# Gate and value products of the dense layer in seven half-width block products for two rounds of three

## The chip, the cores and the metric

The kernel runs on one core of a Trainium2 chip. TensorE multiplies matrices, VectorE, ScalarE and GpSimd work element by element, and DMA queues move data between the main memory and the on-chip memory SBUF. TensorE writes its sums into PSUM, eight banks of 512 fp32 words for each of 128 partitions. The metric is the device time of one execution in microseconds, lower is better.

## The reference

Three layers follow each other: attention with a mask of hash buckets, a mixture of 8 experts with one expert per token, and a gated dense layer. The change touches the last one alone:

```python
n_tokens, d_model, d_ff = (1536, 512, 1536)

rms = np.sqrt(np.mean(x * x, axis=-1, keepdims=True) + 1e-06)
xn = x / rms * rms_g
g = xn @ w_gate
silu = g * (1.0 / (1.0 + np.exp(-g)))
val = xn @ w_val
return (silu * val @ w_out).astype(np.float32)
```

## The kernel before

All large products are made in three bf16 parts: an operand is split into an upper part (its rounded or cut bf16) and a lower part (what is left), and each product is upper by upper, upper by lower and lower by upper. A tile of fp32 words in SBUF serves as its own upper part through its upper halfwords, which are read at a stride of two.

The dense layer runs in 36 steps: three rounds (`ROUNDS`) of 512 tokens (`GROUP`), and in each round 12 steps (`KF2`), one per block of 128 hidden features. Steps count from 0, so round one has steps 0 to 11. In a step `gate_and_value(n)` makes on TensorE the gate block and the value block, [128 features x 512 tokens] each, over a depth of 512 (four chunks of 128): 2 x 4 x 3 = 24 matmuls of 512 columns (L826 to L828), gate into bank 2(n%2), value into bank 2(n%2)+1. So banks 0 to 3 hold two steps in turn, and step n waits for `sv` of step n-2. `project(n-2)` follows: the hidden block of two steps ago times the output weights, four token tiles of three matmuls of 512 columns (L836 to L838) into banks 4 to 7, where they gather over a whole round.

Between the two lies a chain on the other engines, which VectorE writes as follows:

```python
V.tensor_tensor(gp[n % 2][:, :], bank(2 * (n % 2)), inv_at[:, c, :], ALU.mult).then_inc(gp_ready, 1)
dve.wait_ge(sig_ready, n + 1)
V.tensor_tensor(silu[n % 2][:, :], gp[n % 2][:, :], sig[n % 2][:, :], ALU.mult).then_inc(silu_ready, 1)
```

`inv_at` is one over the token's norm, spread over the partitions. ScalarE makes the sigmoid (L1032). VectorE multiplies with the value bank (`sv`, L1346), ScalarE copies `sv` to bf16 (`s_hi`, L882, a line of a helper that all plain copies share), GpSimd subtracts (`s_lo`, L1463). The projection reads `s_hi` and `s_lo`, of which there are three buffers each. The missing factor of the value, the same norm, is applied in `take_rows`, where ScalarE scales the finished output rows (L1025); GpSimd stores them with an indirect DMA. That is done after each round, in steps 13 and 25 and at the end.

In steps 2 and 5 ScalarE scales and GpSimd splits a further group of gate and value weights (L973, L1422), and in round one GpSimd splits the output weights (L1443). Each engine's queue runs in the order in which the code is written, with semaphores between them; there is no scheduler. The last steps are written out: behind the last `gate_and_value` two tiles of the projections 33 and 34, then the wait for the last `s_lo`, then the rest.

Of the kernel before, what the change touches and what calls it, by code (L numbers as in the profile page):

```python
# [55 lines left out]
OUT_AHEAD = 2  # L56

# [77 lines left out]
def tiles_taken(h, t):  # L135

    return T * h + t + 2 + min((h + 1) // 2, PAIRS - 1)

# [9 lines left out]
def build(nc, qk, v, proj, w_router, w1, w2, w_gate, w_val, w_out, rms_g, consts, out):  # L148
# [14 lines left out]
    with ctx:  # L163
# [59 lines left out]
        unused = sb("unused", [P, TT], F32, at)  # L223
        assert at[0] <= nc.sbuf_usable_end, at
# [37 lines left out]
        gp = [sb(f"gp{i}", [P, GROUP], F32, at) for i in range(2)]  # L262
        sig = [sb(f"sig{i}", [P, GROUP], F32, at) for i in range(2)]
        silu = [sb(f"silu{i}", [P, GROUP], F32, at) for i in range(2)]
        sv = [sb(f"sv{i}", [P, GROUP], F32, at) for i in range(2)]
        gram = [ring[c][:, GWORDS:GWORDS + GROUP].rearrange("p (t c) -> p t c", c=P) for c in range(ROUNDS)]
        o_bufs = [x[:, :] for x in o_sb] + [ring[3][:, GWORDS:GWORDS + DM]]
# [18 lines left out]
        w_low = [group_of(x) for x in low]  # L286

# [93 lines left out]
        gv_ready = sem("gv_ready")  # L381
        gp_ready = sem("gp_ready")
        sig_ready = sem("sig_ready")
# [171 lines left out]
        def _(pe):  # L555
# [276 lines left out]

            def project_tile(n, t):
# [27 lines left out]
            for n in range(2, STEPS):  # L861
                gate_and_value(n)
                if n < STEPS - 1:
                    project(n - 2)


            for n in (STEPS - 3, STEPS - 2):
                pe.wait_ge(slo_ready, n + 1)
                for t in range(2):
                    project_tile(n, t)  # L870
            pe.wait_ge(slo_ready, STEPS)
            for t in range(2):
                project_tile(STEPS - 1, t)
            for t in range(2, GT):
                for n in (STEPS - 3, STEPS - 2, STEPS - 1):
                    project_tile(n, t)
# [3 lines left out]
        def _(act):  # L880
# [126 lines left out]
            nc.scalar.activation(unused[:, :], mean[:, :], ACT.Sigmoid)  # L1007
# [8 lines left out]
            def take_rows(c, t):  # L1016
                i = GT * c + t

                if c < ROUNDS - 1:
                    act.wait_ge(projected, GT * (KF2 * c + KF2 - 1) + t + 1)  # L1020
                else:
                    act.wait_ge(finished, t + 1)
                if i >= len(o_bufs):
                    act.wait_ge(o_stored[i % len(o_bufs)], 16 * (i // len(o_bufs)))
                nc.scalar.activation(o_bufs[i % len(o_bufs)], bank(4 + t), ACT.Copy, scale=inv[:, i:i + 1])\  # L1025
                    .then_inc(o_copied, 1)
# [24 lines left out]
        def _(dve):  # L1051
# [282 lines left out]
            for n in range(STEPS):  # L1334
                c = n // KF2
                dve.wait_ge(gate_half, n + 1)
                dve.wait_ge(inv_ready, c + 1)
                V.tensor_tensor(gp[n % 2][:, :], bank(2 * (n % 2)), inv_at[:, c, :], ALU.mult).then_inc(gp_ready, 1)  # L1338
                dve.wait_ge(sig_ready, n + 1)
                V.tensor_tensor(silu[n % 2][:, :], gp[n % 2][:, :], sig[n % 2][:, :], ALU.mult).then_inc(silu_ready, 1)  # L1340
# [5 lines left out]
                V.tensor_tensor(sv[n % 2][:, :], bank(2 * (n % 2) + 1), silu[n % 2][:, :], ALU.mult).then_inc(sv_ready, 1)  # L1346
# [3 lines left out]
        def _(pool):  # L1350
# [103 lines left out]

            def store_rows(c, t):
# [5 lines left out]
            for n in range(STEPS):  # L1461
                pool.wait_ge(shi_ready, n + 1)
                G.tensor_tensor(s_lo[n % 3][:, :], sv[n % 2][:, :], s_hi[n % 3][:, :], ALU.subtract).then_inc(slo_ready, 1)  # L1463
# [32 lines left out]
```

## Time and profile before

| | us |
|---|---|
| median of 3 runs | 714.94 |
| lowest, highest | 713.0, 716.01 |
| the profiled execution | 717.1 |
| its span, first to last instruction | 715.3 |

Busy in the span: TensorE 655.4 us (92%), VectorE 371.5, ScalarE 297.9, GpSimd 405.1. Matmuls are pipelined, so a matmul's own duration (379 ns for 512 columns) is longer than its distance to the next one; for what a row of matmuls costs, the distances between their starts are to be read. The attention takes the time to about 235 us, the experts to about 414, and the dense layer the rest.

### The profile page before, as it was taken

What the parts mean: (1) busy time and instruction counts of PE and PEld (TensorE: products, weight loads), DVE (VectorE), ACT (ScalarE), POOL (GpSimd) and SP (SyncE); (2) the same over time, 40 slices, a digit from 0 to 9 for tenths busy, and PEclk for the clock granted to TensorE, in tenths of its full rate; (3) what the DMA queues carried; (4) which work ended last, traced back from release to release, by engine and by line L of the source; (5) the groups of instructions that cost most, each with busy time, mean ns of one, the idle gap of its engine ahead of it and who ended that gap; (6) DMA issues with size and microseconds to landing.
All of it is one profiled execution on the core that took longest, in us unless ns stands there. A gap on an engine that the chain in (4) does not pass through costs nothing.

```text
span 715.3 us, 14977 instructions
## 1 busy us (share of the span) xinstructions
PE 655.4 (92%) x6360; PEld 425.5 (59%) x6370; DVE 371.5 (52%) x658; ACT 297.9 (42%) x506; POOL 405.1 (57%) x246
## 2 busy tenths in 40 slices
PE   3899999999998459999999789999999999999997
PEld 0256666666676459999999774444444444444442
DVE  6778888898973844554456544332222222222321
ACT  1355655655655036766668844131131111221112
POOL 5278768777878487998889955553131111131112
PEclk8699999999999689999998679999999999999999
DMA  6985576585396169776778990000000000010001
GB/s 169 244 196 121 150 199 124 132 213 117 75 312 262 45 193 255 283 285 238 238 275 299 310 352 4 1 0 1 0 33 27 0 1 1 0 60 1 0 1 59
DMA packets 59427, 94.38 MB, mean 132 GB/s; under 512 B 30208, under 2 KB 34432, under 8 KB 58336
## 3 DMA queue, kind: packets, MB, share of 16 engines
q1 hardware_dynamic: 57440, 87.12, 41.9%
q0 software_dynamic: 1920, 6.31, 2.3%
q8 instruction: 50, 0.82, 0.5%
q14 instruction: 17, 0.14, 0.1%
HBM read 76.98 MB, written 6.30 MB: 116 GB/s over the span
## 4 chain that ended last, share of the span: by engine, by line
PE 76%; DVE 12%; DMA 3%; POOL 3%; ACT 2%; issue 2%; another core or an unknown queue 1%; SPq 1%; POOLq 0%; DVEq 0%; ACTq 0%
PE psum L828 9%; PE psum L826 9%; PE psum L827 9%; PE psum L836 4%; PE psum L837 4%; PE psum L838 4%; PE psum L591 3%; PE psum L755 3%; PE psum L756 3%; PE psum L774 3%; PE psum L757 3%; PE psum L775 3%; PE psum L776 3%; PE psum L605 3%; PE psum L606 2%; DVE psum L1116 2%
## 5 line engine op out<-in xcount | busy, mean ns | idle before, releaser
L1463 POOL TENSOR_TENSOR s_lo<-sv,s_hi 128x512 bf16<-128x512 f32 x36 | 41.7, 1157 | 197.2 <-ACT s_hi L882 197.0
L1381 POOL TENSOR_TENSOR probs_lo<-probs 128x768 bf16<-128x768 f32 x80 | 118.6, 1491 | 61.1 <-ACT probs L920 60.7
L1415 POOL TENSOR_TENSOR low<-ring 128x4096 bf16<-128x4096 f32 x19 | 132.9, 7016 | 16.2 <-DMA ring<-in_moe_w 16.2
L920 ACT ACTIVATE probs<-psum 128x384 f32<-128x384 f32 x192 | 92.6, 490 | 72.6 <-PE psum L606 70.0
L828 PE MATMUL psum<-y,low 128*128 128x512 bf16 x288 | 109.2, 379 | 0.0
L827 PE MATMUL psum<-y,ring 128*128 128x512 bf16 x288 | 109.1, 379 | 0.0
L826 PE MATMUL psum<-y,ring 128*128 128x512 bf16 x288 | 109.1, 379 | 0.0
L1338 DVE TENSOR_TENSOR gp<-psum,inv_at 128x512 f32<-128x512 f32 x36 | 24.9, 691 | 149.7 <-PE psum L828 145.8
L1116 DVE TENSOR_REDUCE psum<-psum 128x1 f32<-128x768 f32 x96 | 88.5, 960 | 15.2 <-PE psum L591 14.5
L1032 ACT ACTIVATE sig<-gp 128x512 f32<-128x512 f32 x36 | 22.7, 630 | 137.7 <-DVE gp L1338 137.7
L774 PE MATMUL psum<-hT,ring 128*128 128x0 bf16 x320 | 68.6, 234 | 4.0 <-POOL low L1415 2.5
L625 PE MATMUL psum<-value,probs 128*128 128x73 bf16 x576 | 69.1, 199 | 3.1 <-POOL probs_lo L1381 2.1
L626 PE MATMUL psum<-value_lo,probs 128*128 128x72 bf16 x576 | 69.0, 195 | 0.0
L627 PE MATMUL psum<-value,probs_lo 128*128 128x73 bf16 x576 | 69.0, 197 | 0.0
L775 PE MATMUL psum<-hT,ring 128*128 128x0 bf16 x320 | 68.5, 234 | 0.0
L776 PE MATMUL psum<-hT,low 128*128 128x0 bf16 x320 | 68.5, 234 | 0.0
L1289 DVE SCALAR_TENSOR_TENSOR hT<-psum,hT 128x512 bf16<-128x512 f32 x80 | 53.7, 689 | 26.8 <-ACT hT L939 25.7
L605 PE MATMUL psum<-head 128*128 128x384 bf16 x192 | 65.0, 338 | 0.8 <-ACT probs L920 0.4
L606 PE MATMUL psum<-head 128*128 128x384 bf16 x192 | 64.2, 334 | 0.0
L625 PEld LDWEIGHTS psum<-value,probs 128*128 128x128 bf16 x576 | 56.0, 97 | 10.8 <-POOL probs_lo L1381 2.9
L591 PE MATMUL psum<-head 96*128 96x384 bf16 x192 | 51.0, 349 | 11.4 <-DVE psum L1116 9.0
L626 PEld LDWEIGHTS psum<-value_lo,probs 128*128 128x128 bf16 x576 | 56.8, 99 | 6.5
(202 smaller groups left out, 1496.8 us busy)
## 6 DMA issues: line engine op xcount, KB each, us to landing
ring<-in_moe_w SPq DMA_DIRECT2D x20, 2048.0 KB, 8.7
pair_in<-in_qk SPq DMA_DIRECT2D x8, 1152.0 KB, 5.8
head<-in_qk SPq DMA_DIRECT2D x16, 384.0 KB
head<-in_qk SPq DMA_DIRECT2D x32, 192.0 KB, 5.3
head<-pair_in SPq DMA_DIRECT2D x32, 192.0 KB, 3.7
value<-in_v SPq DMA_DIRECT2D x16, 192.0 KB, 5.6
ring<-in_moe_w_gate SPq DMA_DIRECT2D x4, 768.0 KB, 9.5
ring<-in_moe_w_val SPq DMA_DIRECT2D x4, 768.0 KB, 10.8
```

What stands on the lines that cost most here:

```text
L625: mm(o, p_hi, value_up[b][:, kt, :], start=(kt == 0), stop=False)
L626: mm(o[:, 0:VW], p_hi, value_lo[b][:, kt, :], start=False, stop=False)
L774: mm(o, w_hi, hh, start=(f == 0), stop=False)
L775: mm(o, w_hi, hl, start=False, stop=False)
L776: last = mm(o, w_lo, hh, start=False, stop=(f == KF - 1))
L826: mm(o, w_up[g][:, a, j, cols], yh, start=(j == 0), stop=False)
L827: mm(o, w_up[g][:, a, j, cols], yl, start=False, stop=False)
L828: last = mm(o, w_low[g][:, a, j, cols], yh, start=False, stop=(j == KD - 1))
L920: nc.scalar.activation(probs[h % 2][:, t, half * HALF:(half + 1) * HALF], bank(ST_BANK + n % 2)[:, 0:HALF], ACT.Exp, scale=SCALE).then_inc ...
L1116: V.reduce_max(row_max[:, t // 2, t % 2:t % 2 + 1], psum[:, first:first + 2, 0:HALF], AX.XY).then_inc(s_free, 1)
L1381: G.tensor_tensor(probs_lo[par][:, t, :], probs[par][:, t, :], probs_up[par][:, t, :], ALU.subtract)\
L1415: G.tensor_tensor(low[k % RING][:, :], ring[k % RING][:, :], upper[k % RING][:, :, 1], ALU.subtract)\
```

## The change

In rounds two and three the product of [gate; value] with the tokens is cut into blocks: two row blocks (gate, value), two halves of the depth (two chunks of 128 each), two halves of the 512 tokens. Eight products of such blocks become seven, by the scheme of Strassen and Winograd: each is a sum of weight blocks times a sum of token blocks, and the four results are sums of products. Round one works as before, except that the silu is one activation (`Silu`) and VectorE's product falls away.

- **TensorE.** `seven_blocks(n)` makes seven products of 2 x 3 matmuls over 256 columns (`SUB`), 42 in all: product 1 (`crossed`) into half of bank 0, products 2 and 3 into bank 1, 4 and 5 into bank 2, 6 and 7 into bank 3. Each step uses the same banks. It waits for copies and joins of the step before (`blocks_copied`, `blocks_taken`). Between steps 11 and 12 the projections 9 and 10 stand together, and none stands between steps 12 and 13.
- **ScalarE.** `copy_blocks(n)` takes product 1 into both middle quarters of `gv` (512 elements), product 2 and product 4 into a quarter each (256). Then silu, `s_hi` and the step's job.
- **VectorE.** `join_blocks(n)` adds and subtracts the other products into `gv`: five instructions of 512, 256, 512, 256 and 512 elements with one operand in PSUM, then `sv`, now with both operands in SBUF.
- **Jobs.** The sums of weights and of tokens are made beforehand, one job a step in steps 1 to 20, through one buffer `mix`: VectorE makes fp32 sums (weights: 512, 512 and 256 elements; tokens, 8 jobs of a quarter each: 512, 512, 128, 256 and 256), ScalarE the upper parts (1024 and 256; 1024), GpSimd the lower parts. The norm is multiplied into the tokens there, so the later rounds' rows of output need no scale. Weights of feature block f are made in step `WEIGHT_AT[f]`, the tokens of rounds two and three in steps `COLUMN_AT`. They are written where their sources stood, or where round one's tokens stood. A job's sums wait for the lower parts of the job before.
- **Rows of output.** A fourth tile of its own takes the place of a piece of the weights' tile. At the end, tile 2 of the projections 33 and 34 stands ahead of the wait for the last `s_lo`.

```diff
+WEIGHT_AT = [1, 3, 5, 7, 9, 10, 11, 12, 14, 16, 18, 20]
+COLUMN_AT = [2, 4, 6, 8, 13, 15, 17, 19]
...
+            def seven_blocks(n):
+
+                c, f, m = n // KF2, n % KF2, n - KF2
+                if c == 1:
+                    pe.wait_ge(mix_low, job_of_weights(f) + 1)
+                if f == 0:
+                    pe.wait_ge(mix_low, job_of_columns(4 * c - 1) + 1)
+                left, right = slice(0, SUB), slice(SUB, GROUP)
+                if m:
+                    pe.wait_ge(blocks_copied, COPIES * (m - 1) + 1)
+                else:
+                    pe.wait_ge(sv_ready, KF2 - 1)
+                crossed(bank(0)[:, left], c, f, B_CROSS).then_inc(blocks_ready, 1)
+                if m:
+                    pe.wait_ge(blocks_copied, COPIES * (m - 1) + 2)
+                    pe.wait_ge(blocks_taken, TAKES * (m - 1) + 1)
+                plain(bank(1)[:, left], c, f, 1, B_STEP)
+                mixed(bank(1)[:, right], c, f, C_STEP, B_UPPER).then_inc(blocks_ready, 1)
...
-            for n in range(2, STEPS):
+            for n in range(2, KF2):
                 gate_and_value(n)
+                project(n - 2)
+            project(KF2 - 2)
+            seven_blocks(KF2)
+            for n in range(KF2 + 1, STEPS):
+                seven_blocks(n)
                 if n < STEPS - 1:
                     project(n - 2)
...
             for n in range(STEPS):
-                act.wait_ge(gp_ready, n + 1)
+                if n < KF2:
+                    act.wait_ge(gp_ready, n + 1)
+                else:
+                    copy_blocks(n)
+                    act.wait_ge(blocks_taken, TAKES * (n - KF2 + 1))
                 if n >= 2:
-                    act.wait_ge(silu_ready, n - 1)
-                nc.scalar.activation(sig[n % 2][:, :], gp[n % 2][:, :], ACT.Sigmoid).then_inc(sig_ready, 1)
+                    act.wait_ge(sv_ready, n - 1)
+                nc.scalar.activation(silu[n % 2][:, :], gp[n % 2], ACT.Silu).then_inc(silu_ready, 1)
...
-                copy(s_hi[n % 3][:, :], sv[n % 2][:, :]).then_inc(shi_ready, 1)
+                copy(s_hi[n % 3][:, :], sv[n % 2]).then_inc(shi_ready, 1)
                 if n in SPLIT_AT:
                     scale_group(SPLIT_AT.index(n) + 2)
+                if n in WEIGHT_AT:
+                    weights_high(WEIGHT_AT.index(n))
+                if n in COLUMN_AT:
+                    columns_high(COLUMN_AT.index(n))
...
+            def mix_weights(f):
+
+                g, cols = f // GF, slice((f % GF) * P, (f % GF + 1) * P)
+                if job_of_weights(f):
+                    dve.wait_ge(mix_low, job_of_weights(f))
+                dve.wait_ge(w_scaled, KD * (g + 1))
+                w = group_of(ring[g])[:, :, :, cols]
+                V.tensor_tensor(mix[:, 0:4 * P].rearrange("p (a j c) -> p a j c", a=2, j=2), w[:, :, 0:2, :], w[:, :, 2:4, :], ALU.add)
...
+            for n in range(STEPS):
+                if n < KF2:
+                    gate_and_value(n)
+                else:
+                    join_blocks(n)
+                if n in WEIGHT_AT:
+                    mix_weights(WEIGHT_AT.index(n))
+                if n in COLUMN_AT:
+                    mix_columns(COLUMN_AT.index(n))
...
+                if n in WEIGHT_AT:
+                    weights_low(WEIGHT_AT.index(n))
+                if n in COLUMN_AT:
+                    columns_low(COLUMN_AT.index(n))
```

ScalarE's queue from step 12 to step 14, before: a sigmoid and an `s_hi` per step, and in step 13 the four rows of output.

```order
L1032 ACTIVATE sig_161<-gp_159 128x512
L882 ACTIVATE s_hi_149<-sv_165 128x512
L1032 ACTIVATE sig_162<-gp_160 128x512
L882 ACTIVATE s_hi_150<-sv_166 128x512
L1025 ACTIVATE o_sb_155<-psum,inv 128x512
```

The same place after the change, from the silu of step 12 to the copies of step 14 (L999 is the helper for copies; `ring`, `low` and `y` hold the sums):

```order
L1186 ACTIVATE silu_162<-gv_160 128x512
L999 ACTIVATE s_hi_150<-gv_160 128x512
L999 ACTIVATE ring_107<-mix 128x4x256
L999 ACTIVATE low_111<-mix 128x2x128
L999 ACTIVATE gv_161<-psum 128x512
L999 ACTIVATE gv_161<-psum 128x256 x2
L1186 ACTIVATE silu_163<-gv_161 128x512
L999 ACTIVATE s_hi_151<-gv_161 128x512
L999 ACTIVATE y<-mix 128x4x2x128
L1143 ACTIVATE o_sb_156<-psum,inv 128x512
```

The upper parts of the step's job stand behind `s_hi` and ahead of the next step's copies, and in step 13 the rows of output stand behind the job. VectorE's queue in one of these steps, before: three instructions per step.

```order
L1338 TENSOR_TENSOR gp_160<-psum,inv_at 128x512
L1340 TENSOR_TENSOR silu_164<-gp_160,sig_162 128x512
L1346 TENSOR_TENSOR sv_166<-psum,silu_164 128x512
```

And after the change, in step 13 (a job of tokens) and, by its first lines, in every step from 12 on:

```order
L1544 TENSOR_TENSOR gv_161<-gv_161,psum 128x512
L1547 TENSOR_TENSOR gv_161<-gv_161,psum 128x256
L1549 TENSOR_TENSOR gv_161<-gv_161,psum 128x512
L1551 TENSOR_TENSOR gv_161<-gv_161,psum 128x256
L1553 TENSOR_TENSOR gv_161<-gv_161,psum 128x512
L1555 TENSOR_TENSOR gv_161<-gv_161,silu_163 128x512
L1516 TENSOR_TENSOR mix<-y 128x512
L1517 TENSOR_TENSOR mix<-mix,inv_at 128x512
L1519 TENSOR_TENSOR mix<-mix 128x128
L1520 TENSOR_TENSOR mix<-mix 128x256
```

Three instructions became six with five of them joins, and a job's sums stand between `sv` and the next step's joins.

## Rows read from the trace of the kernel before

**Rows 1.** Windows: busy PE, PEld, DVE, ACT, POOL (instructions), granted clock, DMA share, GB/s.
```profile
449.00:701.50 252.50, 252.50 (x1160) 112.55 (x1159) 69.62 (x98) 48.86 (x77) 61.86 (x54) 1.00 0.02 9
```

**Rows 2.** Timeline of TensorE in one step: start, duration, engine, line, operation.
```profile
563.28 0.38 PE L826 MATMUL psum<-y,ring 128*128 128x512 bf16 x1
...
568.46 0.39 PE L836 MATMUL psum<-wo,s_hi 128*128 128x512 bf16 x1
...
571.13 0.38 PE L826 MATMUL psum<-y,ring 128*128 128x512 bf16 x1
```

**Rows 3.** Timeline of the other engines in the same step.
```profile
568.76 0.69 DVE L1346 TENSOR_TENSOR sv<-psum,silu 128x512 f32<-128x512 f32 x1 [0.61 <-PE psum L828]
569.49 0.63 ACT L882 ACTIVATE s_hi<-sv 128x512 bf16<-128x512 f32 x1 [2.06 <-DVE sv L1346]
570.19 1.16 POOL L1463 TENSOR_TENSOR s_lo<-sv,s_hi 128x512 bf16<-128x512 f32 x1 [6.69 <-ACT s_hi L882]
```

**Rows 4.** Timeline of TensorE, token norms of 128 columns, thirteen starts.
```profile
420.78 0.22 PE L801 MATMUL psum<-y 128*128 128x128 bf16 x1
...
421.45 0.22 PE L801 MATMUL psum<-y 128*128 128x128 bf16 x1
```

**Rows 5.** Timeline of the weight loads in the expert stage, neighbours.
```profile
382.02 0.10 PEld L774 LDWEIGHTS psum<-hT,ring 128*128 128x128 bf16 x1
382.10 0.10 PEld L775 LDWEIGHTS psum<-hT,ring 128*128 128x128 bf16 x1
```

**Rows 6.** Groups by shape: count, busy us, mean ns, then idle time before.
```profile
L882 ACT ACTIVATE y<-psum 128x512 f32 x36 | 20.4, 592 | 16.2 <-PE psum L776 15.9
L920 ACT ACTIVATE probs<-psum 128x384 f32<-128x384 f32 x192 | 92.6, 490 | 72.6 <-PE psum L606 70.0
L882 ACT ACTIVATE s_hi<-sv 128x512 bf16<-128x512 f32 x36 | 22.7, 630 | 74.1 <-DVE sv L1346 74.1
L882 ACT ACTIVATE even_window<-xT 128x1536 bf16 x2 | 3.0, 1486 | 0.0
L1346 DVE TENSOR_TENSOR sv<-psum,silu 128x512 f32<-128x512 f32 x36 | 24.9, 692 | 19.6 <-PE psum L828 19.5
L1150 DVE TENSOR_TENSOR x_head<-psum,rden 128x384 f32<-128x384 f32 x16 | 8.9, 558 | 0.5
L1331 DVE TENSOR_TENSOR ring<-cst,inv 128x512 f32<-128x512 f32 x3 | 1.9, 686 | 0.0
L1463 POOL TENSOR_TENSOR s_lo<-sv,s_hi 128x512 bf16<-128x512 f32 x36 | 41.7, 1157 | 197.2 <-ACT s_hi L882 197.0
L1415 POOL TENSOR_TENSOR low<-ring 128x4096 bf16<-128x4096 f32 x19 | 132.9, 7016 | 16.2 <-DMA ring<-in_moe_w 16.2
```

**Rows 7.** Timeline: VectorE with both operands in SBUF beside GpSimd.
```profile
60.89 0.96 DVE L1183 TENSOR_TENSOR probs_lo<-probs 128x768 bf16<-128x768 f32 x1
61.76 2.33 DVE L1093 TENSOR_TENSOR pair_in<-pair_in 128x768 bf16<-128x768 f32 x1
...
61.49 1.68 POOL L1381 TENSOR_TENSOR probs_lo<-probs 128x768 bf16<-128x768 f32 x1 [1.15 <-ACT probs L920]
...
191.87 2.34 DVE L1093 TENSOR_TENSOR pair_in<-pair_in 128x768 bf16<-128x768 f32 x1
...
439.69 0.69 DVE L1346 TENSOR_TENSOR sv<-psum,silu 128x512 f32<-128x512 f32 x1
...
449.76 1.87 DVE L1340 TENSOR_TENSOR silu<-gp,sig 128x512 f32<-128x512 f32 x1 [0.70 <-ACT sig L1032]
```

**Rows 8.** Timeline of TensorE in the tail, around the wait for the last s_lo.
```profile
704.31 0.38 PE L838 MATMUL psum<-wo_lo,s_hi 128*128 128x512 bf16 x1
704.79 0.40 PE L836 MATMUL psum<-wo,s_hi 128*128 128x512 bf16 x1
```

**Rows 9.** Waits of TensorE in the expert stage; windows, columns as in rows 1.
```profile
PE psum L774 <- POOL low L1415: 2.5, 1, 2.5
...
388.00:392.00 4.00, 2.88 (x57) 2.64 (x58) 4.00 (x8) 3.74 (x8) 4.00 (x1) 0.59 0.90 328
272.00:276.00 4.00, 2.50 (x32) 2.36 (x31) 1.31 (x2) 0.60 (x2) 4.00 (x2) 1.00 1.14 206
276.00:280.00 4.00, 4.00 (x51) 4.00 (x49) 0.69 (x1) 4.00 (x3) 4.00 (x1) 1.00 1.10 150
```

More of the change, by code:

```diff
@@ L137, in tiles_taken, with job_of_weights, job_of_columns @@
     return T * h + t + 2 + min((h + 1) // 2, PAIRS - 1)
+def job_of_weights(f):
+    return f + sum(n < WEIGHT_AT[f] for n in COLUMN_AT)
+def job_of_columns(i):
+    return i + sum(n < COLUMN_AT[i] for n in WEIGHT_AT)
 def item_of_hidden(u):
@@ L286, in build, with mixed_high, mixed_low, cross @@
         w_low = [group_of(x) for x in low]
+        mixed_rows = [x[:, 0:GWORDS].bitcast(BF16).rearrange("p (r c) -> p r c", r=2 * KD)[:, 2:6, :] for x in ring]
+        low_rows = [x[:, 0:GWORDS].rearrange("p (r c) -> p r c", r=2 * KD) for x in low]
+        def mixed_high(f):
+            g, i = f // GF, f % GF
+            return mixed_rows[g][:, :, i * 2 * P:(i + 1) * 2 * P]
+        def mixed_low(f):
+            g, i = f // GF, f % GF
+            tail = low[g][:, GWORDS:ITEM] if i == 2 else ring[g][:, GWORDS + 512 * i:GWORDS + 512 * (i + 1)].bitcast(BF16)
+            return tail.rearrange("p (r c) -> p r c", r=4)
+        def cross(f, part):
+            g, i = f // GF, f % GF
+            return low_rows[g][:, 2 + 2 * part:4 + 2 * part, i * P:(i + 1) * P]
+        def columns_of(c, jj, part):
+            first = c * GROUP if part else (NTOK if c == 1 else 0)
+            return y[:, :, jj::2, first:first + GROUP].rearrange("p a k c -> p (a k) c")\
+                .rearrange("p m (h c) -> p m h c", h=2)
         psum = ctx.enter_context(nc.psum_tensor("psum", [P, 8, 512], F32))
@@ L831, in gate_and_value, with block, mixed @@
                         spread(0)
+            def block(o, jj, high, low_part, c, operand, first, last):
+                x_hi, x_lo = (columns_of(c, jj, part)[:, operand // 2, operand % 2, :] for part in range(2))
+                mm(o, high, x_hi, start=first, stop=False)
+                mm(o, high, x_lo, start=False, stop=False)
+                return mm(o, low_part, x_hi, start=False, stop=last)
+            def mixed(o, c, f, unit, operand):
+                for jj in range(2):
+                    cols = slice(jj * P, (jj + 1) * P)
+                    last = block(o, jj, mixed_high(f)[:, unit, cols], mixed_low(f)[:, unit, cols], c, operand, jj == 0, jj == 1)
+                return last
@@ new lines, in crossed, with plain @@
+            def crossed(o, c, f, operand):
+                for jj in range(2):
+                    last = block(o, jj, cross(f, 0)[:, jj, :], cross(f, 1)[:, jj, :], c, operand, jj == 0, jj == 1)
+                return last
+            def plain(o, c, f, a, operand):
+                g, cols = f // GF, slice((f % GF) * P, (f % GF + 1) * P)
+                for jj in range(2):
+                    j = 2 * a + jj
+                    last = block(o, jj, w_up[g][:, a, j, cols], w_low[g][:, a, j, cols], c, operand, jj == 0, jj == 1)
+                return last
@@ L1006, in _ @@
             nc.scalar.activation(root[:, :], mean[:, :], ACT.Sqrt).then_inc(root_ready, 1)
-            nc.scalar.activation(unused[:, :], mean[:, :], ACT.Sigmoid)
+            nc.scalar.activation(unused[:, :], mean[:, :], ACT.Silu)
             def take_spread(c):
@@ L1336, in _, with gate_and_value @@
+            def gate_and_value(n):
                 dve.wait_ge(gate_half, n + 1)
[L1337 to L1340, printed above, removed]
+                dve.wait_ge(inv_ready, 1)
+                if n >= 2:
+                    dve.wait_ge(silu_ready, n - 1)
+                V.tensor_tensor(gp[n % 2], bank(2 * (n % 2)), inv_at[:, 0, :], ALU.mult).then_inc(gp_ready, 1)
@@ L1462, in _ @@
                 pool.wait_ge(shi_ready, n + 1)
-                G.tensor_tensor(s_lo[n % 3][:, :], sv[n % 2][:, :], s_hi[n % 3][:, :], ALU.subtract).then_inc(slo_ready, 1)
+                G.tensor_tensor(s_lo[n % 3][:, :], sv[n % 2], s_hi[n % 3][:, :], ALU.subtract).then_inc(slo_ready, 1)
                 if n + OUT_AHEAD < KF2:
```

126 lines of the change are left out of this document (113 added, 13 removed).

## The prediction

> **What bounds the kernel now.** I read the profile in this order: the page's busy times, then the time slices of the dense layer, then one step as a timeline on each engine, then the tail. From 449 to 701.5 us TensorE is busy for the whole stretch at a granted clock of 1.00, while VectorE is busy 69.6 us, ScalarE 48.9 and GpSimd 61.9 of the 252.5 [rows 1]. One step lasts 7.85 us: the 24 gate and value matmuls from 563.28 to 568.46, so 5.18 us or 215.7 ns each, then the 12 projection matmuls to 571.13, 2.67 us or 222.3 ns each [rows 2]. The other engines follow with a chain (gp, sig, silu, sv, s_hi, s_lo) that ends at 571.35, far ahead of the projection two steps later that reads it [rows 3]. So every nanosecond off TensorE in this stage counts, as long as the others stay behind it. That condition is the whole question here.
>
> **TensorE's gain.** A step of rounds two and three replaces 24 matmuls over 512 columns by 42 over 256 (seven products, two row blocks, three parts). The trace has no matmul of 256 columns at a known width. It has 512 columns at 215.7 ns, and the token norms with 128 columns: twelve from 420.78 to 421.45, 55.8 ns each [rows 4]. The line through both gives 109.2 ns. Weight loads last 98 ns and might stand out at that spacing, but in the expert stage matmuls with such loads follow each other every 83 ns [rows 5], so they are hidden. Bounds: 106.7 (half of 213.3, the columns alone) and 112. A step then takes 42 x 0.1092 = 4.59 us instead of 5.18, with the projection 7.25 instead of 7.85. Over 24 steps that is **-14.2 us**.
>
> **What the others now do in a step.** Before, the ring of buffers had two sets of banks; now each step uses banks 0 to 3, and the next step may write them only as they are emptied. In a step of rounds two and three the work of ScalarE and VectorE is one chain: copy 1 to 3, joins 1 to 5, silu, sv, and only then, in a step with a job, the job's sums on VectorE and its upper parts on ScalarE. ScalarE's queue is in order, so the next step's copy 1 stands behind those upper parts, and with it the joins, and behind these TensorE's next products. I call the time from copy 1 of a step to copy 1 of the next the ring.
>
> Prices. ScalarE from PSUM: 592 ns for 512 and 490 for 384, so 380 for 256; from SBUF 630 for 512, 1486 for 1536, so 1.06 us for 1024 and 0.42 for 256. VectorE: 692 for 512, 558 for 384, so 424 for 256. GpSimd: 1157 for 512 and 7016 for 4096, so 1.99 us for 1024 and 0.74 for 256 [rows 6]. The next instruction of an engine that need not wait starts 0.09 us before the one ahead ends: three of 686 ns take 1.90 us [rows 6]. From engine to engine 0.04 us passes, to GpSimd 0.07 [rows 3].
>
> A ring with a job of weights: copies until join 1 can start 0.50 + 0.38 + 0.04 = 0.92; joins 0.60 + 0.33 + 0.60 + 0.33 + 0.69 = 2.55; silu and sv 0.67 + 0.73 = 1.40; sums 2.52 (below); upper parts 0.04 + 0.97 + 0.33 = 1.34. Together **8.73 us**. A job of columns has sums of 3.23 and one upper part of 0.97 + 0.04: **9.11 us**. Without a job the ring is 5.5. TensorE's step is 7.25: job steps are bound by the ring, the others by TensorE.
>
> The sums' price is the term to watch. By themselves the three sums of a weights job end 1.54 us after sv. But s_hi ends 0.67 after sv, and s_lo on GpSimd wants to start at 0.74, inside the second sum. What happens then is in the trace: at 60.89 VectorE runs a tensor_tensor on SBUF, GpSimd's op at 61.49 starts in the middle of it, and VectorE's next, 0.96 us by itself, takes 2.33 us, until 0.92 after GpSimd is done. The silu product, 0.69 us by itself, takes 1.87 us beside GpSimd, while `sv`, which reads PSUM, takes 0.69 beside it [rows 7]. So the third sum waits for s_lo: it starts at 2.10 and ends at 2.52. In a columns job two of the sums are linked and three wait likewise: 3.23 instead of 2.35.
>
> On this the Trainium skill speaks against the change ("GPSIMD Engine Reference", section Specifications): GpSimd shares its SBUF interfaces with VectorE, and contends with VectorE's instructions that have two SBUF inputs. The five or three new sums of each job are just such instructions, the joins are not. The trace agrees, by the 2.33 us above; with this rule the sum comes to +3.6 us, without it to the -6.2 of rival (1).
>
> **Following the queues.** Time 0 is TensorE's first product of step 12. Jobs are in steps 12 to 20 (weights 12, 14, 16, 18, 20; columns 13, 15, 17, 19). Copy 1 of step 12 starts at 3.8, not at 1.0 when its product is there: steps 9, 10 and 11 all have a job of weights, each job's sums wait until GpSimd has left the one buffer (upper parts 1.4, lower parts 2.7, s_lo and the sums held as above), which is a loop of nearly the 7.85 us of a step, so step 11's upper parts end at 3.8. In step 13 ScalarE also takes four rows of output, 4 x 0.59 = 2.4 us behind the job. Copy 1 of step 21 thus starts at 3.8 + 5 x 8.73 + 4 x 9.11 + 2.4 = 86.3. TensorE's product 1 of step 22 waits for that copy's end, 86.9. By itself TensorE would be there at 4.59 + 9 x 7.25 = 69.9 (steps 12 and 13 follow without a projection between). It has waited **17.0 us**, and 0.4 more for join 1 within step 22. Most of it falls at one place: 4.2 us before projection 12, which needs the banks of the first output rows; the rest is 1.5 or 1.8 in each of steps 14 and 16 to 22. From step 23 on the ring of 5.5 is hidden again.
>
> **Tail.** Before, the last s_lo was covered by 12 matmuls and TensorE waited 0.25 us, from 704.54 to 704.79 [rows 8]. Now 18 matmuls, 4.0 us, cover a chain of 0.3 + joins 0.33 + 0.69 + silu 0.67 + sv 0.73 + s_hi 0.67 + s_lo 1.27 = 4.7: a wait of 0.7, **+0.4 us**. From the last matmul to the end nothing changes.
>
> **At nothing** I set: Silu in place of Sigmoid and the product taken from VectorE in round one (one activation for one, 630 ns; VectorE has slack there); the sums of steps 1 to 8, hidden behind a 7.85 us step, with 10 us between an s_lo and the projection that reads it [rows 3]; the larger tile of output, the same four stores.
>
> **Sum.** -14.2 + 17.4 + 0.4 = +3.6 us. The profiled execution took 717.1 us with its 715.3 span, so it would take 720.7; the median of the three runs, 714.94, becomes **718.6**, 0.5% slower. A difference below about 0.5% (3.6 us) can't be told from none by such measurements, so the forecast lies on that border, on the slow side.
>
> **Rivals.** (1) GpSimd does not hold the sums, or s_lo comes late enough to queue behind all of them. Then the rings are 7.74 and 8.23, the start is 1.0, copy 1 of step 21 starts at 76.4 and the wait is 7.2 + 0.4: -14.2 + 7.6 + 0.4 = -6.2, **708.8**, faster. For it: the arrival of s_lo at 0.74 is only some tenths from the gap between sums. Against it: the same op in the same place lasts 2.33 or 2.34 us in six instances from 61.76 to 191.87 [rows 7]. (2) The ring never catches TensorE, since the copies and joins overlap more than I allow, or VectorE's sums take less: -14.2 + 0.4, **701.1**. It needs 1.5 us less in each ring than the rows give. (3) The ring is longer still: with 0.4 us more for each job's sums the loop of steps 9 to 11 passes 7.85 us, the start moves to 7.7, and the wait grows by 7.7 us: **726.3**. For it: operands of four dimensions and rows of 128 or 256 elements, which the rows above don't show. The clock belongs here: after an idle stretch of 2.5 us it fell to a mean of 0.59 at 388, most of that window at 1.2 GHz of the two levels; after 1.5 us at 272 it stayed at 1.00 [rows 9], and 4.2 us before projection 12 may lower it; but TensorE then has some 4 us of room before the ring needs it, so I price that at 0 to 2. (4) Matmuls of 256 columns cost 130 ns, not 109, for instance through the upper halves read at a stride: the ring hides it in the job steps, the total is +15.7, **730.6**. Against it the 83 ns of the expert stage. That the block products don't save columns at all is excluded by their count.
>
> **Chances.** The forecast 0.50, rival (1) 0.20, (2) 0.07, (3) 0.18, (4) 0.05. The forecast's own spread is 713 to 724, since a tenth in each of nine rings is 0.9 us and the start lies between 1 and 5. The range takes in (1) and most of (3): 706 to 729. Faster by over 0.5% (below 711.4): 0.26; within: 0.30; slower (above 718.5): 0.44.
>
> **What would show it.** In the changed trace: matmuls of 256 columns every 109 ns; in steps 12 to 20 a period of 8.7 to 9.1 us and TensorE idle for ScalarE's copies or VectorE's joins, 17 us in all, with one wait of some 4 us for the output rows; in steps 23 to 34 a period of 7.25; the third sum of a weights job at 1.0 us or more where 0.42 is its own time. If the sums end 1.6 us after sv, rival (1) holds; if TensorE has no wait in round two, (2). Wrong altogether would be a wait in round three, or a period above 7.4 there.

## The result

| | before | after |
|---|---|---|
| median, runs of the same chip | 713.19 us (7 runs) | 720.3 us (7 runs) |
| lowest, highest | 711.62, 716.01 | 718.8, 721.65 |
| ratio | | 1.0096, 95% interval 1.0082 to 1.011 |
| the profiled execution, its span | 717.1, 715.3 | 720.3, 718.5 |

The changed kernel is 1.0% slower, by more than the 0.5% that such a measurement can tell. A second comparison, on another chip, gave 1.0083 (1.0058 to 1.0108), and the kernel before measured against itself there 1.0005 (0.999 to 1.0019). The median forecast was 718.6. That forecast started from 714.94, the median of three runs, where the seven give 713.19: against the kernel before it said +3.6 us and the measured difference is +7.1, so part of the nearness of 718.6 to 720.3 is luck.

First the stretch of rows 1 again, in the changed kernel, windows with busy PE, PEld, DVE, ACT, POOL (instructions), granted clock, DMA share, GB/s:

```profile
449.00:701.50 252.50, 236.69 (x1530) 150.93 (x1556) 146.27 (x226) 98.04 (x176) 115.04 (x84) 0.99 0.03 9
```

TensorE is no longer busy throughout: 236.7 of 252.5 us where it was 252.5 [rows 1]. VectorE's and ScalarE's work has doubled, 69.6 to 146.3 and 48.9 to 98.0. The view of TensorE's waits from 420 to 716 us says for whom it stood (us in total, times, longest):

```profile
PE psum L888 <- ACT gv L999: 7.8, 7, 1.9
PE psum L947 <- ACT o_sb L1143: 4.4, 1, 4.4
PE psum L888 <- DVE gv L1544: 2.0, 8, 0.3
PE psum L946 <- POOL s_lo L1700: 0.5, 1, 0.5
```

The kernel before has no row at all in this view. Each of these waits is counted from the modelled end of the last matmul, some 0.16 us after the next could have started, so I count by distances between starts. TensorE's timeline at products (256 columns) and at the one long wait:

```profile
516.53 0.27 PE L888 MATMUL psum<-y,low 128*128 128x256 bf16 x1
516.64 0.27 PE L889 MATMUL psum<-y,low 128*128 128x256 bf16 x1
...
531.83 0.27 PE L888 MATMUL psum<-y,low 128*128 128x256 bf16 x1 [0.86 <-ACT gv L999]
...
541.34 0.63 PE L947 MATMUL psum<-wo,s_lo 128*128 128x512 bf16 x1 [4.36 <-ACT o_sb L1143]
...
546.03 0.42 PE L888 MATMUL psum<-y,low 128*128 128x256 bf16 x1
...
605.07 0.27 PE L888 MATMUL psum<-y,low 128*128 128x256 bf16 x1 [0.86 <-ACT gv L999]
...
612.73 0.27 PE L888 MATMUL psum<-y,low 128*128 128x256 bf16 x1
...
619.98 0.27 PE L888 MATMUL psum<-y,low 128*128 128x256 bf16 x1
```

The first products of steps 12, 14, 15, 22, 23 and 24 are shown. From step 23 to 24 7.25 us pass, instead of the 7.85 of before [rows 2]: here the gain is whole. From step 12 to 22 it is 88.54 us, where 4.59 + 9 x 7.25 = 69.84 is TensorE's own work, and 0.4 more is lost inside step 22: 19.1 us lost, all between steps 12 and 23. Some 16.8 us of it TensorE stands still; the rest goes in matmuls at the lower clock (below).

To compare kernels I take the dense layer by itself, from the start of its first gate matmul to the start of the last projection matmul. Before, 424.80 to 709.92: 285.1 us. After, 422.46 to 712.78: 290.3 us (the record of the first matmul is missing; the second stands at 422.67, 0.21 behind). The second profiles of both kernels gave 285.1 and 290.4. So the layer takes 5.2 us longer; its beginning alone moves between 422.5 and 428.4 us over the traces of all kernels here, which is why spans are a poorer measure. Behind the last matmul a further 0.4 us is lost:

```profile
708.98 0.40 PE L946 MATMUL psum<-wo,s_hi 128*128 128x512 bf16 x1 [0.50 <-POOL s_lo L1700]
...
710.73 0.98 POOL L1695 DMA_INDIRECT out<-o_sb,gi  x1 [1.81 <-ACT o_sb L999]
...
712.02 0.96 POOL L1695 DMA_INDIRECT out<-o_sb,gi  x1 [0.30 <-ACT o_sb L999]
...
712.78 0.38 PE L948 MATMUL psum<-wo_lo,s_hi 128*128 128x512 bf16 x1
...
713.28 0.96 POOL L1695 DMA_INDIRECT out<-o_sb,gi  x1 [0.30 <-issue]
714.55 0.96 POOL L1695 DMA_INDIRECT out<-o_sb,gi  x1 [0.30 <-issue]
```

The four stores stand behind one another, 1.27 us each, since tiles 0, 1 and 2 now end close together; the last starts 1.77 us after the last matmul, before it was 1.38. Together 5.6 us, which agrees with the second ratio (5.9 us) and lies just below the interval of the first (5.8 to 7.8 us of 713.19); what the first shows beyond it I can't place in the dense layer (see the end of the section on the prediction).

**The ring in one step.** Step 12 on ScalarE, VectorE and GpSimd, from its three copies to the first copy of step 13:

```profile
522.42 1.12 ACT L999 ACTIVATE gv<-psum 128x512 f32<-128x512 f32 x3
523.38 0.69 DVE L1544 TENSOR_TENSOR gv<-gv,psum 128x512 f32<-128x512 f32 x1 [2.26 <-ACT gv L999]
...
525.95 0.63 ACT L1186 ACTIVATE silu<-gv 128x512 f32<-128x512 f32 x1 [2.41 <-DVE gv L1553]
526.62 0.69 DVE L1555 TENSOR_TENSOR gv<-gv,silu 128x512 f32<-128x512 f32 x1 [0.70 <-ACT silu L1186]
527.23 0.68 DVE L1499 TENSOR_TENSOR mix<-ring 128x512 f32<-128x512 f32 x1
527.34 0.63 ACT L999 ACTIVATE s_hi<-gv 128x512 bf16<-128x512 f32 x1 [0.76 <-DVE gv L1555]
527.83 0.68 DVE L1500 TENSOR_TENSOR mix<-ring 128x512 f32<-128x512 f32 x1
528.05 1.48 POOL L1700 TENSOR_TENSOR s_lo<-gv,s_hi 128x512 bf16<-128x512 f32 x1 [2.70 <-ACT s_hi L999]
528.43 1.38 DVE L1501 TENSOR_TENSOR mix<-ring 128x256 f32<-128x256 f32 x1
529.84 1.06 ACT L999 ACTIVATE ring<-mix 128x1024 bf16<-128x1024 f32 x1 [1.87 <-DVE mix L1501]
530.80 0.40 ACT L999 ACTIVATE low<-mix 128x256 bf16<-128x256 f32 x1
531.11 0.58 ACT L999 ACTIVATE gv<-psum 128x512 f32<-128x512 f32 x1
```

Copy to copy 531.11 - 522.42 = 8.69 us (forecast 8.73). The third sum (L1501), 0.41 us by itself, takes 1.38 and ends 0.28 us behind s_lo; and s_lo itself takes 1.48 instead of 1.15, since it begins inside the second sum. Copy 1 of step 21 starts at 604.34, so the nine rings took 81.9 us against 82.5 in the forecast.

**The clock** after the long wait (windows, columns as above):

```profile
536.00:540.00 4.00, 0.98 (x10) 0.64 (x7) 3.08 (x5) 1.45 (x2) 1.60 (x1) 0.97 0.00 0
540.00:544.00 4.00, 2.66 (x7) 1.12 (x9) 0.59 (x1) 3.58 (x8) 3.23 (x3) 0.50 0.02 4
544.00:548.00 4.00, 4.00 (x22) 2.31 (x21) 3.30 (x8) 1.26 (x2) 2.77 (x3) 0.67 0.53 204
548.00:552.00 4.00, 3.94 (x33) 3.08 (x32) 1.83 (x2) 2.13 (x5) 2.16 (x2) 1.00 0.15 58
```

TensorE comes back at 1.2 GHz (0.50) and stays there for the eleven matmuls from 541.34 to 546.03, 4.69 us instead of 2.45. It changes nothing in the sum: copies and joins of steps 15 and 16 are not earlier, so the next two steps have nearly no wait for them (the distances to steps 16 and 17 are 7.54 and 7.33) and the ring catches TensorE again at step 18. Two later runs bear this out: small_group and small_wo (below) both wait 4.4 us here, the eleven matmuls then take 4.69 and 3.56 us, and the layer takes 286.9 us in both.

### The profile page after: what moved, and what is told of

Same layout as the page of the kernel before. It is cut to its first block, busy times and chain, and to the rows that moved or that the text cites. A ratio compares the mean times of both kernels' runs of the same rounds, so it can differ in the third digit from the quotient of the medians.

```text
span 718.5 us, 16200 instructions
## 1 busy us (share of the span) xinstructions
PE 645.0 (90%) x6760; PEld 468.0 (65%) x6802; DVE 455.3 (63%) x794; ACT 349.3 (49%) x610; POOL 462.1 (64%) x278
## 4 chain that ended last, share of the span: by engine, by line
PE 52%; DVE 22%; POOL 10%; issue 7%; ACT 6%; DMA 3%; SPq 1%; POOLq 0%; DVEq 0%; ACTq 0%
PE psum L643 3%; PE psum L888 3%; PE psum L826 3%; PE psum L827 3%; PE psum L828 3%; PE psum L890 3%; PE psum L889 3%; PE psum L657 3%; PE psum L658 2%; PE psum L807 2%; PE psum L808 2%; PE psum L809 2%; DVE psum L1274 2%; PE psum L677 2%; PE psum L947 2%
## 5 line engine op out<-in xcount | busy, mean ns | idle before, releaser
L1700 POOL TENSOR_TENSOR s_lo<-gv,s_hi 128x512 bf16<-128x512 f32 x36 | 45.4, 1261 | 108.0 <-ACT s_hi L999 108.0
L888 PE MATMUL psum<-y,ring 128*128 128x256 bf16 x288 | 78.5, 272 | 2.0 <-DVE gv L1544 2.0
L889 PE MATMUL psum<-y,ring 128*128 128x256 bf16 x288 | 78.5, 272 | 0.0
L826 PE MATMUL psum<-hT,ring 128*128 128x0 bf16 x320 | 69.9, 238 | 7.7 <-POOL low L1634 7.7
L827 PE MATMUL psum<-hT,ring 128*128 128x0 bf16 x320 | 69.9, 238 | 0.0
L1456 DVE TENSOR_TENSOR y<-psum,y 128x512 f32 (+1 forms) x40 | 26.4, 688 | 57.1 <-ACT y L999 57.1
L947 PE MATMUL psum<-wo,s_lo 128*128 128x512 bf16 x142 | 55.9, 394 | 5.8 <-ACT o_sb L1143 4.4
L1056 ACT ACTIVATE hT<-psum 128x512 bf16<-128x512 f32 x80 | 46.8, 600 | 22.6 <-PE psum L809 22.3
```

Source lines behind the costliest of these rows:

```text
L826: mm(o, w_hi, hh, start=(f == 0), stop=False)
L827: mm(o, w_hi, hl, start=False, stop=False)
L888: mm(o, high, x_hi, start=first, stop=False)
L889: mm(o, high, x_lo, start=False, stop=False)
```

## The experiments

The theory: the loss is the ring's. In steps 12 to 20 ScalarE's queue holds the next step's copies behind the job's upper parts, these behind the sums, and the last sum behind s_lo. Rivals: that the hold by s_lo is not what lengthens the sums; that the matmuls or the joins themselves are too dear; and, once the start proved later than forecast, that the loop of jobs in steps 9 to 11 is long by itself.

**no_late_jobs.** The jobs of steps 12 to 20 are left out on all engines (VectorE's part is shown).

```diff
-                c, f, m = n // KF2, n % KF2, n - KF2
+                c, f, m = 1, n % KF2 % 7, n - KF2
...
-                if n in WEIGHT_AT:
+                if n in WEIGHT_AT and n < KF2:
                     mix_weights(WEIGHT_AT.index(n))
```

> Left out: the jobs of steps 12 to 20, so that the later products read the sums of the first seven feature blocks and of round two again. Ring theory: the ring of copies, joins, silu and sv is then 5.5 us in every step of rounds two and three, TensorE waits for nobody there but for the last s_lo, and the time is that of the change less its 14 us of waits and the 1 us of the start: 703 to 706. Rival, that the block products themselves or the copies and joins cost the time: it stays above 712.

Measured: 706.75 us against 716.9 before, ratio 0.9844 (0.9816 to 0.9872). The dense layer takes 273.7 us, 11.4 less than before, with one wait for a copy (1.9 us, step 13) and the 0.5 of the tail. So the products, copies and joins are no hindrance: -14.3 for TensorE's gain, +2.5 for the copy and a join in step 13 (behind the job of step 11, which stays), +0.4 in the tail is -11.4. All of the loss in rounds two and three comes with the jobs.

The expected ranges of the first four runs were set against the first chip's times. On this chip the kernel before takes 716.9 us, 3.7 more, and three of the medians lie above their ranges: 706.75 (703 to 706), 720.27 (716 to 718) and 706.7 (702 to 706). The ratios and the dense layer are what I go by.

**small_slo.** s_lo on one column in steps 3 to 20 (its lower parts are left out, the instruction and its semaphores stay).

```diff
+                some = slice(0, 1) if 3 <= n <= 20 else slice(0, GROUP)
-                G.tensor_tensor(s_lo[n % 3][:, :], sv[n % 2], s_hi[n % 3][:, :], ALU.subtract).then_inc(slo_ready, 1)
+                G.tensor_tensor(s_lo[n % 3][:, some], sv[n % 2][:, some], s_hi[n % 3][:, some], ALU.subtract).then_inc(slo_ready, 1)
```

> Left out: in steps 3 to 20 GpSimd's s_lo works on one column of 512, the jobs stay. If GpSimd's hold on the shared path to SBUF makes the third sum wait, the third sum of a weights job takes 0.41 us again instead of 1.38, the rings shrink from 8.7 and 9.0 to 7.8 and 8.2, and the waits of TensorE fall from 14 to some 6 us: 708 to 711. If the sums were slow for another reason, the third sum stays at 1.38 and the time at 720.

Measured: 710.91 us, ratio 0.9924 (0.99 to 0.9948), dense layer 278.8 us: 11.6 less than the change. The sums of step 12 in its timeline (VectorE):

```profile
525.93 0.69 DVE L1499 TENSOR_TENSOR mix<-ring 128x512 f32<-128x512 f32 x1
526.53 0.69 DVE L1500 TENSOR_TENSOR mix<-ring 128x512 f32<-128x512 f32 x1
527.13 0.42 DVE L1501 TENSOR_TENSOR mix<-ring 128x256 f32<-128x256 f32 x1
```

The third sum is back at its own 0.42 us. Nothing on VectorE was changed, so the 1.38 us was the hold by s_lo, and s_lo at its full width, in nine rings and in the loop of round one, decides the sign of the change. The run takes both away at once: copy 1 of step 12 starts 0.9 us behind its product instead of 5.9, and the later rings with a job take 7.73 and 8.21 us instead of 8.69 and 9.04. As an estimate from these, nine such rings are worth 8.1 us by themselves, more than the 5.2 that the change loses in the layer. What part of the earlier start is the hold and what part is GpSimd's shorter queue this run can't tell.

**rows_first.** In step 13 the four rows of output ahead of the job's upper parts on ScalarE; the whole computation.

```diff
+                if n % KF2 == 1 and n > KF2:
+                    for t in range(GT):
+                        take_rows(n // KF2 - 1, t)
                 if n in WEIGHT_AT:
                     weights_high(WEIGHT_AT.index(n))
                 if n in COLUMN_AT:
                     columns_high(COLUMN_AT.index(n))
-                if n % KF2 == 1 and n > KF2:
...
```

> One order changed on ScalarE: in step 13 the four output rows stand ahead of the upper parts of the job, not behind. They then run while VectorE makes the job's sums. By the queues followed the wait of 4.4 us ahead of projection 12 falls below 1, but steps 14 to 16 get waits of 1 to 1.5 us that they did not have, so only 3.3 us is gained: 716 to 718. If the row copies were the whole cause of that wait and nothing stood behind them, 4.4 us would be gained.

Measured: 720.27 us, ratio 1.0056 (1.0034 to 1.0078), dense layer 287.1, 3.2 less than the change. In the change ScalarE is idle for 2.52 us ahead of this job's upper parts; here the rows fill that time, and the wait before projection 12 falls from 4.4 to 0.6 us. The ring from step 13 to 14 takes 9.05 us instead of 11.31, and the next one 7.73 instead of 8.72, for a reason that I had not foreseen:

```profile
546.70 0.42 DVE L1501 TENSOR_TENSOR mix<-ring 128x256 f32<-128x256 f32 x1
...
548.31 1.17 POOL L1700 TENSOR_TENSOR s_lo<-gv,s_hi 128x512 bf16<-128x512 f32 x1
```

In step 14 s_lo stands behind the four stores in GpSimd's queue and comes after the sums, and the third sum takes its own 0.42 us. This is the hold taken away in a whole computation, with s_lo as wide as ever. The granted clock stays at 1.00. The waits for copies grow (9.7 us in 9 instead of 7.8 in 7): without the long stop the ring catches TensorE already at step 15.

**defer_one.** The whole computation. From step 11 on, a job's upper parts stand behind the three copies of the next step on ScalarE, and its lower parts ahead of that step's s_lo on GpSimd.

```diff
                     copy_blocks(n)
+                    upper_job(n - 1)
                     act.wait_ge(blocks_taken, TAKES * (n - KF2 + 1))
...
+                if n >= KF2:
+                    lower_job(n - 1)
                 pool.wait_ge(shi_ready, n + 1)
```

> The whole computation. From step 11 on ScalarE makes the upper parts of a job only after the three copies of the next step, and GpSimd the lower parts ahead of that step's s_lo. The upper parts and the sums then no longer stand between a step's chain and the next step's copies: the ring on VectorE is joins 2.55, silu and sv 1.40, sums 2.4 to 3.2, some 6.4 to 7.2 us, below TensorE's 7.25. Ring theory: waits of 2 to 3 us in all, 16 us less than the change: 702 to 706. Rival (the sums' own load on VectorE and GpSimd is the cause): above 712.

Measured: 706.7 us against 716.9, ratio 0.9857 (0.984 to 0.9873), dense layer 274.5: 15.8 less than the change and 10.6 less than before. TensorE's waits:

```profile
PE psum L888 <- DVE gv L1550: 1.7, 2, 1.1
PE psum L947 <- ACT o_sb L1143: 0.9, 1, 0.9
PE psum L946 <- POOL s_lo L1715: 0.5, 1, 0.5
```

and the queues in its step 12, from the copies of step 13 on:

```profile
527.96 1.13 ACT L999 ACTIVATE gv<-psum 128x512 f32<-128x512 f32 x3
528.13 1.53 POOL L1715 TENSOR_TENSOR s_lo<-gv,s_hi 128x512 bf16<-128x512 f32 x1 [0.21 <-ACT s_hi L999]
528.56 1.64 DVE L1506 TENSOR_TENSOR mix<-ring 128x512 f32<-128x512 f32 x1
530.13 0.41 DVE L1507 TENSOR_TENSOR mix<-ring 128x256 f32<-128x256 f32 x1
530.46 0.68 DVE L1550 TENSOR_TENSOR gv<-gv,psum 128x512 f32<-128x512 f32 x1
530.57 1.06 ACT L999 ACTIVATE ring<-mix 128x1024 bf16<-128x1024 f32 x1 [1.49 <-DVE mix L1507]
```

The hold by s_lo is still there (L1506, 1.64 instead of 0.69 us). But the copies no longer wait for the sums, and the upper parts run beside the joins: of the 8.7 us ring the 1.34 of the upper parts and most of the copies' 0.92 are gone. From join 1 to the next join 1 it is 7.31 us here (523.15 to 530.46), and from step 15 on 6.36 with a job of weights and 7.96 with one of tokens, 7.16 on average against TensorE's 7.25, so TensorE no longer waits from step 18 on. Before that it loses 3.3 us, in part since the product `sv`, 0.69 us by itself, now runs beside GpSimd's lower parts and takes 1.0 us there, once even 3.12 (the lower part in question ran from 542.20 to 544.34):

```profile
541.78 3.12 DVE L1561 TENSOR_TENSOR gv<-gv,silu 128x512 f32<-128x512 f32 x1 [0.70 <-ACT silu L1194]
```

This version beats both kernels.

**after_again, before_again, tail_as_before, defer_tail.** On a second chip: the two kernels once more, and the old order of the last projections in the change and in defer_one.

```diff
-            for n in (STEPS - 3, STEPS - 2):
-                project_tile(n, 2)
             pe.wait_ge(slo_ready, STEPS)
             for t in range(2):
                 project_tile(STEPS - 1, t)
-            project_tile(STEPS - 1, 2)
-            for n in (STEPS - 3, STEPS - 2, STEPS - 1):
-                project_tile(n, 3)
+            for t in range(2, GT):
+                for n in (STEPS - 3, STEPS - 2, STEPS - 1):
+                    project_tile(n, t)
```

> The changed kernel once more, beside the kernel before on the same chip. The traces put the change at 3.9 us in the dense layer and 0.4 at the last store, 4.3 us; the first comparison of medians gave 6.9. Theory A: the stages ahead vary by some us between executions and chips, so the two differ by noise: the ratio here lies between 1.004 and 1.009 (3 to 6.5 us). Theory B: something outside the dense layer is slower with the change: the ratio is 1.009 or more again and the span ahead of the first gate matmul is longer than before by 2 us or more.

> The kernel before, unchanged, for its trace. Theory A: the dense layer again takes 285.1 us within 0.3 from the first gate matmul to the last projection matmul, its start moves by 1 to 4 us against 424.8, and the ratio is 1. Theory B: the dense layer itself varies by us.

> The change with the end of TensorE's order undone: the wait for the last s_lo stands behind 12 matmuls again, not 18. TensorE's wait there grows from 0.5 to 1.8 us, so the last matmul comes 1.3 later. If the last of the four stores is held up by the three ahead of it, as the trace of the change suggests (1.8 us from the last matmul's start to it, where before it was 1.4), that goes, and 0.9 us is lost; if not, 1.3.

> The whole computation: upper and lower parts of the jobs deferred behind the next step's copies, with the end of TensorE's order as before. Against the same without the old end (ratio 0.986 to before) 0.9 us more by the theory of the stores, 1.3 without it: ratio 0.987 or 0.988.

Measured, against 716.09 us before: after_again 723.3 us, ratio 1.0083 (1.0058 to 1.0108), dense layer 290.4; before_again 716.88, 1.0005 (0.999 to 1.0019), 285.1; tail_as_before 723.57, 1.0091 (1.0067 to 1.0115), 291.6; defer_tail 708.46, 0.9885 (0.9863 to 0.9906), 275.8. (The 289.0 and 3.9 us that these expectations name for the change were read without the first matmuls of the layer; counted in full they are 290.3 and 5.2.) The old order costs TensorE 1.3 us more in both pairs (291.6 - 290.4, 275.8 - 274.5), the wait for the last s_lo being 1.8 instead of 0.5. Of that it gives 0.5 back. The last matmul and the last store of tail_as_before:

```profile
717.21 0.38 PE L948 MATMUL psum<-wo_lo,s_hi 128*128 128x512 bf16 x1
...
718.49 0.95 POOL L1693 DMA_INDIRECT out<-o_sb,gi  x1 [1.04 <-ACT o_sb L997]
```

are 1.28 us apart instead of 1.78 in after_again, since here the tiles end one after another and the stores don't queue. Net the new order is worth 0.8 us in the traces; the medians, 0.3 apart with intervals of 1.7 us to either side, can't show it.

**small_group and small_wo.** For the late start: the copies of step 12 began 5.9 us behind TensorE's first product (516.53 to 522.42), not 3.8. The trace of the change shows, in round one:

```profile
472.46 6.37 POOL L1641 TENSOR_TENSOR low<-ring 128x768 bf16<-128x768 f32 x4
...
481.57 1.63 DVE L1516 TENSOR_TENSOR mix<-y 128x512 f32<-128x512 bf16 x1 [4.28 <-POOL low L1680]
...
490.01 1.49 POOL L1662 TENSOR_TENSOR wo_lo<-wo 128x512 bf16<-128x512 f32 x1
...
490.52 1.52 DVE L1500 TENSOR_TENSOR mix<-ring 128x512 f32<-128x512 f32 x1
```

GpSimd's split of the last group of weights in step 5 makes the job of step 6 late: VectorE stands for 4.3 us ahead of its first sum, which starts 59.1 us into the layer, where it is 55.2 without the split (small_group, below). And in each step to 9 the split of output weights (L1662) holds a second sum of the job. I took either away, by one column in place of all (the lower parts are left out; in small_wo the projection reads another block's).

```diff
+                    some = slice(0, 1) if n == 3 else slice(0, GF * P)
-                    last = G.tensor_tensor(w_low[i][:, :, j, :], group_of(ring[i])[:, :, j, :], w_up[i][:, :, j, :],
+                    last = G.tensor_tensor(w_low[i][:, :, j, some], group_of(ring[i])[:, :, j, some], w_up[i][:, :, j, some],
```

```diff
+                some = slice(0, 1) if f >= 6 else slice(0, DM)
-                G.tensor_tensor(wo_lo[:, f, :], wo[:, f, :], wo_up[:, f, :, 1], ALU.subtract).then_inc(wo_split, 1)
+                G.tensor_tensor(wo_lo[:, f, some], wo[:, f, some], wo_up[:, f, some, 1], ALU.subtract).then_inc(wo_split, 1)
```

> The change with one thing taken away: the last split of a group of weights on GpSimd (step 5, four instructions that take 6.37 us) works on one column instead of 384, so the lower parts of those weights are left out. Theory: the first copy of step 12 starts late (5.9 us behind its product, where 3.8 had been forecast) because this split made the jobs late from step 6 on, by about 3.2 us at step 7, and the loop of sums, upper parts and lower parts, 7.4 and 7.7 us a step against TensorE's 7.85, makes up only 0.3 us a step. Without it the sums of step 11 start right behind sv and the copy starts at 2.8 to 3.3; each us goes straight into the waits of rounds two and three, so the dense layer takes 287.3 to 287.9 instead of 290.3 us, ratio near 1.0045. Rival: the loop of steps 9 to 11 by itself sets the start. Then the copy stays at 5.9 and the dense layer at 290.3, ratio 1.008 to 1.0095.

> The change with one thing taken away: GpSimd's split of the output weights works on one column from feature block 6 on (steps 4 to 9; the projection reads another block's lower part, in as many matmuls). Theory: in steps 5 to 9 of the change this instruction, 1.48 us in GpSimd's queue, holds the second sum of the job (1.41 to 1.52 us instead of 0.69), which the forecast of the loop had left out. Without it the loop is some 1.0 to 1.5 us shorter a step, the lateness of 3.2 us at step 7 is gone by step 10, and the copy of step 12 starts at 2.8 to 3.3 instead of 5.9: dense layer 287.3 to 287.9 instead of 290.3 us, ratio near 1.0045. Rival: the split only fills a gap in GpSimd's queue, and the loop is bound by the sums and the upper and lower parts. Then the copy stays near 5.9 and the ratio at 1.008 to 1.0095.

Measured, against 717.09 us before: small_group 720.13, ratio 1.0049 (1.003 to 1.0068); small_wo 719.69, 1.0042 (1.0028 to 1.0055); dense layer 286.9 in both, 3.4 less than the change. The layer is 0.4 us below what I had expected. TensorE's first product and ScalarE's first copy of step 12 in small_group:

```profile
518.63 0.27 PE L888 MATMUL psum<-y,low 128*128 128x256 bf16 x1
...
520.63 0.85 ACT L999 ACTIVATE gv<-psum 128x512 f32<-128x512 f32 x2
```

The copy starts 2.0 us behind the product, in small_wo 1.2 (519.11 to 520.31), earlier than I expected of either. In both the wait for a copy at step 13 is gone. So the rival falls: the loop of steps 9 to 11 by itself leaves a start of 2 us at most. It takes both splits to make it 5.9: the one in step 5 brings the lateness, the ones of the output weights keep it, since with their hold the loop (7.4 and 7.7 us) gains only tenths on 7.85 in each of the steps to 9. In small_wo the loop takes 6.7 or 6.8 us in steps 6 to 11.

## Why the prediction was right, and where it was not

- **TensorE's gain** of 14.2 us: right, 14.3. 109 ns between 256-column matmuls, 7.25 us a step in round three, and no wait there from step 23 on.
- **The hold of the sums by s_lo**: right, and the place on which the sign hung; small_slo shows it. Rival (1) would have been the outcome without it: forecast -6.2 us, and small_slo's layer and stores give -5.9. (Its 76.4 us for copy 1 of step 21 is more than its terms as written, 1.0 + 5 x 7.74 + 4 x 8.23 + 2.4 = 75.0. In small_slo it is 76.25, since the first ring takes 9.23: with an early start its copies wait for their products.)
- **The rings**: right, 81.9 us for nine against 82.5.
- **Where the waits lie**: right in the main. 4.4 us before projection 12 (forecast 4.2); 1.4 or 1.8 in each of steps 18 to 22, 1.0 before step 14. Not forecast were 2.5 us at step 13 (2.0 for a copy, 0.4 for a join), which the late start brought. Steps 16 and 17 had nearly none, since the slower clock had used that time up; as forecast it cost nothing, with 2.2 us lost on TensorE inside the room.
- **The rows on the clock** were misread. The wait of 2.5 us for L1415 [rows 9] stands ahead of 409.58, where the granted clock had been near 0.50 since 402. Ahead of the window of 0.59 TensorE had stood for 1.1 us only, from 387.7 to 388.76. So the rows gave no price by the length of a stop; the 0 to 2 us held all the same, by the room that the ring leaves.
- **The start** was the term that was mis-sized: 5.9 us instead of 3.8, outside the 1 to 5 that I had allowed it. The step read "steps 9, 10 and 11 all have a job of weights ... which is a loop of nearly the 7.85 us". Such a loop of 7.4 to 7.7 us there was, but only up to step 10, and by things that the step left out: the hold by the output weights' split in steps 5 to 9. From step 10 to 11, with the forecast's own parts alone, it took 6.83, and would have caught up. The lateness itself came from the 6.37 us split of step 5, also left out. small_group and small_wo show it. (The lower parts, priced at 1.99 + 0.74 us, took 2.13 + 0.67.) The wait is 19.1 us instead of 17.4: +2.1 by the start, -0.6 by the rings, the rest rounding of the single waits.
- **"At nothing: the sums of steps 1 to 8, hidden behind a 7.85 us step"**: wrong in the same way. They were hidden from TensorE in round one, but the lateness they passed on was not hidden in round two.
- **Tail**: the wait for the last s_lo was 0.65 by the starts (708.11 + 0.22 to 708.98; the view's 0.50 counts from the modelled end), forecast 0.7, before 0.25: right. **"From the last matmul to the end nothing changes"** was wrong by 0.4 us: the stores now queue on GpSimd. Together 0.8 instead of 0.4.
- **Sum**: -14.3 + 19.1 + 0.8 = +5.6 us, forecast +3.6. Of the three outcomes the slow side, the likeliest, came true, though the forecast itself lay on its border.

Left open is what lies outside the layer. The first comparison is 0 to 2 us above 5.6. In all ten comparisons of a changed kernel the ratio gives 0.0 to 2.0 us more than the difference of the dense layers, 1.0 on average, of which the stores explain 0.4 in eight of them; the kernel before against itself gives 0.4. The interval of each is 1 to 2 us to either side, but all lie on one side, so some half a us more may be real. The traces don't place it: the layer begins at 424.8 and 423.5 in the two of the kernel before and anywhere from 422.5 to 428.4 in the ten of the changed ones. (In after_again it begins 2.9 us later than in before_again, as theory B asked; in the first pair it is 2.3 earlier.)

## What to carry to other kernels

Where a faster engine uses one set of buffers in place of two, the time from one step's first read to the next step's is a ring; sum it over all in-order queues that it passes, with what stands in them only by the order of the code. Here the upper parts of a job for steps to come stood ahead of the copies TensorE waited for, and moving them behind turned +5.2 us in the dense layer into -10.6. And a helper's load that is hidden in one stage can still hand its lateness to the next: look at how early its last job is done, not only at who waits for it there.

## What the runs showed of the hardware

- The hold between VectorE and GpSimd goes by whole instructions and both ways. VectorE's third sum ran until 0.28 us behind the end of s_lo, and s_lo, begun 0.22 us into a second sum of 0.68, took 1.48 us instead of 1.15. I had priced the first, not the second. The Trainium skill has this as an exclusive lock, held for a full instruction, on the port pair that the two share ("SBUF — State Buffer", section "SBUF: two separate sides"); the trace agrees, by the 1.38 and the 1.48 us. It also shows who goes first: s_lo, waiting since 528.05, went ahead of the third sum, whose record starts at 528.43, though that stood next in VectorE's own queue.
- The joins, with one operand in PSUM, kept their own time beside GpSimd: L1544 took 687 ns on average over 24, and the one at 523.38 its 0.69 us in the middle of a lower part of 2.13 us (522.59 to 524.72).
- TensorE stood still for 4.4 us and came back at 1.2 GHz, 0.50 in the window after it. After 0.6 us in rows_first and 0.9 us in defer_one at the same place the windows stayed at 1.00; after 2.8 us in small_slo the first two matmuls still came at 2.4 GHz, and those from 538.55 to 541.53 at 1.2 GHz (0.63 us each instead of 0.39).
